# Attention in front of two feed-forward networks: contiguous copies, scores of one head on 64 rows, first fills shared by two engines

## What is computed

```python
scores = scale * np.matmul(q, k.transpose(0, 1, 3, 2))
mask_local = (rel >= 0) & (rel < stride)                       # heads 0 to 3
mask_strided = (rel >= 0) & (pos[None, :] % stride == pos[:, None] % stride)   # heads 4 to 7
scores = np.where(masks, scores, -1e9); scores -= scores.max(-1, keepdims=True)
attn = np.exp(scores); attn /= attn.sum(-1, keepdims=True) + 1e-9
x = np.matmul(attn, v)                                         # then as 2304 x 512
...
for e in range(E):
    out += P[:, e:e + 1] * (np.maximum(x @ w1[e], 0.0) @ w2[e])
...
h = x @ w_in; return np.where(h > 0, h, np.exp(np.minimum(h, 0)) - 1) @ w_out
```

## Time and profile before

| | us |
|---|---|
| median of 3 runs | 2070.46 |
| lowest, highest | 2066.57, 2079.49 |
| the profiled execution | 2081.29 |
| its span | 2079.5 |
| end of attention, where the networks begin to fill PE | 189.8 |

### The profile page before, as it was taken

The page is one execution under the profiler, slowest core; times in us unless marked ns, Lnnn a source line. Parts: engine busy times, 40 slices in busy tenths (PEclk is TensorE's granted clock), DMA queues, the critical chain, the costliest instruction groups (busy, mean ns, idle before and its releaser), DMA issues. The chain is left out here.

```text
span 2079.5 us, 29859 instructions
## 1 busy us (share of the span) xinstructions
PE 2037.2 (98%) x10611; PEld 1841.7 (89%) x10611; DVE 1430.5 (69%) x2456; ACT 931.8 (45%) x1708; POOL 1163.4 (56%) x1519
## 2 busy tenths in 40 slices
PE   6889999999999999999999999999999999999999
PEld 5878999999999999999999998999999999998988
DVE  3664776666666776666666778776666666678876
ACT  5884334333333333333333377533333333477775
POOL 2344665545545565555555657675555554557653
PEclk8997999999999999999999999999999999999999
DMA  7431222212222222222212222322221222222221
GB/s 149 91 76 43 70 62 72 71 62 71 71 62 72 71 61 62 81 61 63 80 61 63 80 61 61 96 77 62 70 73 61 71 72 61 72 67 66 92 71 52
DMA packets 159555, 147.69 MB, mean 71 GB/s; under 512 B 64688, under 2 KB 126384, under 8 KB 159408
## 3 DMA queue, kind: packets, MB, share of 16 engines
q1 hardware_dynamic: 159408, 145.79, 24.3%
HBM read 141.05 MB, written 4.72 MB: 70 GB/s over the span
## 5 line engine op out<-in xcount | busy, mean ns | idle before, releaser
L486 POOL TENSOR_TENSOR w_lo<-w_raw,w_hi 128x256 fp32r<-128x256 f32 x480 | 354.1, 768 | 752.3 <-ACT w_hi L822 752.3
L1088 DVE SCALAR_TENSOR_TENSOR acc<-psum,prob_eps,acc 128x512 f32<-128x512 f32 x516 | 386.9, 750 | 276.0 <-PE psum L695 270.1
L693 PE MATMUL psum<-w_hi,h_hi 128*128 128x512 f32 x1440 | 563.2, 391 | 0.6 <-issue 0.6
L695 PE MATMUL psum<-w_hi,h_lo 128*128 128x512 f32 x1440 | 563.4, 391 | 0.0
L694 PE MATMUL psum<-w_lo,h_hi 128*128 128x512 f32 x1440 | 561.4, 390 | 0.0
L634 PE MATMUL psum<-x_hi_a,w_hi 128*128 128x384 f32 x1296 | 439.2, 339 | 4.1 <-DVE c L1055 3.4
L637 PE MATMUL psum<-x_hi_a,w_lo 128*128 128x384 f32 x1296 | 439.0, 339 | 0.0
L636 PE MATMUL psum<-x_lo_a,w_hi 128*128 128x384 f32 x1296 | 437.6, 338 | 0.0
L479 POOL TENSOR_TENSOR w_lo<-s_tmp,w_hi 128x256 fp32r<-128x256 f32 x480 | 358.3, 777 | 0.0
L695 PEld LDWEIGHTS psum<-w_hi,h_lo 128*128 128x128 f32 x1440 | 270.3, 188 | 58.0
L693 PEld LDWEIGHTS psum<-w_hi,h_hi 128*128 128x128 f32 x1440 | 270.3, 188 | 43.9 <-issue 0.9
(11 more groups left out here) (115 smaller groups left out, 2800.5 us busy)
## 6 DMA issues: line engine op xcount, KB each, us to landing
w_raw<-in_moe_w_dram SPq DMA_DIRECT2D x192, 512.0 KB, 3.6
w_raw<-in_moe_w_in_dram SPq DMA_DIRECT2D x24, 512.0 KB, 3.4
w_raw<-in_moe_w_out_dram SPq DMA_DIRECT2D x24, 512.0 KB, 3.7
v_l<-in_v_dram SPq DMA_DIRECT2D x24, 128.0 KB, 3.5
out_dram<-acc SPq DMA_DIRECT2D x2, 1536.0 KB, 6.8
raw_l_q<-in_q_dram SPq DMA_DIRECT2D x16, 144.0 KB, 3.3
raw_l_k<-in_k_dram SPq DMA_DIRECT2D x16, 144.0 KB, 3.6
raw_s_q<-in_q_dram SPq DMA_DIRECT2D x16, 144.0 KB
```

The costliest lines, as they stand in the source:

```text
L486: pool.tensor_tensor(w2_lo[n % 2][piece], w2_raw[piece], w2_hi[n % 2][piece].bitcast(f32), ALU.subtract).then_inc(w2_lo_s, 1)
L693: pe.matmul(dst, h_hi[:, i, kk, js], w2_hi[s][:, i, :], start=(i == 0), stop=False)
L695: mm = pe.matmul(dst, h_lo[:, i, kk, js], w2_hi[s][:, i, :], start=False, stop=(i == 1))
L1088: ins = dve.scalar_tensor_tensor(a, y, 1.0 if bare else gate_of(n, j), a, ALU.mult, ALU.add)
```

## The change

- `load_qk` of the local heads: two issues for each of q and k instead of four, one for each half of the tokens, all four heads in one. The tokens of a half are now consecutive, so a fill holds 288 neighbouring tokens.
- The transposes of a fill and of a strided context write their columns into PSUM in token order, so with gaps (`fill_ps`, `x_ps`), and the copies out of it are contiguous (`fill_views`, `x_views`). Each fill is one copy, each group has one x copy.
- `kT` loses its zero halves, and its two memsets. Scores: one matmul for each head, on its own 64 partitions, in the order of heads 0, 1, 2, 3; the heads of the lower partitions write bank 0, those of the upper ones bank 1. The two banks now belong to one group, and the scores of g wait for the mask of g-1. The heads stand in the order 0, 2, 1, 3 from the scores to the context (`HEADS`).
- The first eight fills: ACT copies the even ones, DVE the odd ones (`fill_dve`).
- ACT takes one exponential of a column of `ones` before its first wait for a fill, which brings the table of exponentials in.

```diff
-            kT = [sb(f"kT_{kind}", [P, NH // 2, 2, S], f32, att) for kind in "ls"]
+            kT = [sb(f"kT_{kind}", [P, NH // 2, S], f32, att) for kind in "ls"]
...
+        HEADS = (0, 2, 1, 3)
+
         def score_ps(g):
-            return bank(SC + g % 2).rearrange("p (h w) -> p h w", h=NH)
+            return bank(SC, 2).rearrange("p (h w) -> p h w", h=NH)
...
                 for n, src in enumerate((q, k)):
-                    view = src.rearrange("b h (p j) d -> p j b h d", j=run)
-                    for h in range(NH):
-                        sp.dma_start(raw[n][:, :, h * D:(h + 1) * D],
-                                     view[:, :, b, kind * NH + h, :]).then_inc(qk_in[kind][n], 16)
+                    if kind == 0:
+
+                        tokens = src.rearrange("b h (f p j) d -> f p j b h d", f=2, j=run // 2)
+                        for f in range(2):
+                            sp.dma_start(raw[n][:, f * (run // 2):(f + 1) * (run // 2), :]
+                                         .rearrange("p j (h d) -> p j h d", h=NH),
+                                         tokens[f, :, :, b, 0:NH, :]).then_inc(qk_in[kind][n], 16)
+                    else:
+                        tokens = src.rearrange("b h (p j) d -> p j b h d", j=run)
+                        for h in range(NH):
+                            sp.dma_start(raw[n][:, :, h * D:(h + 1) * D],
+                                         tokens[:, :, b, NH + h, :]).then_inc(qk_in[kind][n], 16)
...
-            for m in (kT[0], kT[1]):
-                pool.memset(m[:, :, :, :], 0.0).then_inc(pads_made, 1)
...
+        def fill_views(kind, f):
             which, pair, half = f // 4, (f // 2) % 2, f % 2
             src = bank(FILL + f % 2)[:, 0:FILL_COLS]
+            dst = (qT, kT)[which][kind][:, pair, :]
+            if kind == 0:
+                return dst[:, half * FILL_COLS:(half + 1) * FILL_COLS], src
+            n = FILL_COLS // RES_RUNS
+            return (dst.rearrange("p (a c) -> p a c", a=RES_RUNS)[:, :, half * n:(half + 1) * n],
+                    src.rearrange("p (a c) -> p a c", a=RES_RUNS))
+
+        def fill_read(eng, i):
+
+            if 0 <= i < FILLS and i % 2:
+                eng.wait_ge(fill_dve, i // 2 + 1)
+            elif i >= 0:
+                eng.wait_ge(fill_out, i // 2 + 1 if i < FILLS else i + 1 - FILLS // 2)
+
+        def fill_ps(kind, f, j):
+
+
+            src = bank(FILL + f % 2)[:, 0:FILL_COLS]
+            if kind == 0:
+                return src.rearrange("p (c j) -> p j c", j=L_RUN // 2)[:, j, :]
+            return src.rearrange("p (a j m) -> p j m a", a=RES_RUNS, m=PER_RES)[:, j, :, :]
+
+        def x_ps(g, c):
+
+            cols_c = bank(XT)[:, c * P:c * P + rows_of(g)]
+            return cols_c if g < L_TILES else cols_c.rearrange("p (m r) -> p r m", m=PER_RES)
+
+        def x_views(b, g):
             r = rows_of(g)
+            src = bank(XT)[:, 0:2 * P].rearrange("p (c w) -> p c w", c=2)[:, :, 0:r]
+            if g < L_TILES:
+                return xT[:, 0:2, b * S + g * L_ROWS:b * S + g * L_ROWS + L_ROWS], src
+            r0, n_res = (g - L_TILES) * RES_TILE, r // PER_RES
+            return (xT[:, 2:4, b * S:(b + 1) * S].rearrange("p c (m r) -> p c m r", r=STRIDE)[:, :, :, r0:r0 + n_res],
+                    src.rearrange("p c (m r) -> p c m r", m=PER_RES))
...
-                wait(pe, masked, b * GROUPS + g - (1 if g else 0))
+                wait(pe, masked, b * GROUPS + g)
                 q0, k0 = cols(g)
                 r, w = rows_of(g), keys_of(g)
-                for pair in range(NH // 2):
-                    mm = pe.matmul(score_ps(g)[0:r, 2 * pair:2 * pair + 2, 0:w], qT[kind][:, pair, q0:q0 + r],
-                                   kT[kind][:, pair, :, k0:k0 + w], start=True, stop=True)
+                for i in (0, 2, 1, 3):
+                    pair, o = divmod(HEADS[i], 2)
+                    rows = slice(o * D, (o + 1) * D)
+                    mm = pe.matmul(score_ps(g)[0:r, i, 0:w], qT[kind][rows, pair, q0:q0 + r],
+                                   kT[kind][rows, pair, k0:k0 + w], start=True, stop=True)
...
                 for c in range(2):
-                    mm = pe.transpose(bank(XT)[:, c * P:c * P + r], ctx_n[g % 2][0:r, 2 * c:2 * c + 2, :],
-                                      ident[0:r, 0:r])
+                    mm = pe.transpose(x_ps(g, c), ctx_n[g % 2][0:r, 2 * c:2 * c + 2, :], ident[0:r, 0:r])
...
-            act.wait_ge(pads_made, 2)
-            for f in range(FILLS):
+
+            act.wait_ge(ones_made, 1)
+            act.activation(top_neg[:, :], ones[:, 0:1], ACT.Exp)
+            for f in range(0, FILLS, 2):
                 fill_copy(0, 0, f)
...
+            for f in range(1, FILLS, 2):
+                dve.wait_ge(filled, f + 1)
+                dve.tensor_copy(*fill_views(0, f)).then_inc(fill_dve, 1)
```

More of the change, by code:

```diff
@@ L207, in build @@
         fill_out = sem("fill_out")
+        fill_dve = sem("fill_dve")
         scored = sem("scored")
@@ L509, in _ @@
                         make_t(PHASE[v_] + 1, t)
-        def fill_copies(kind, f):
+        def fill_views(kind, f):
             which, pair, half = f // 4, (f // 2) % 2, f % 2
             src = bank(FILL + f % 2)[:, 0:FILL_COLS]
[L514 to L526, removed]
@@ L528, in x_copies @@
-        def x_copies(b, g):
-            r = rows_of(g)
[L530 to L537, removed]
+            dst = (qT, kT)[which][kind][:, pair, :]
@@ L543, in fill @@
                 if f % (FILLS // 2) == 0:
-                    pe.wait_ge(qk_in[kind][which], (NH * 16) * (b + 1))
+                    pe.wait_ge(qk_in[kind][which], (2, NH)[kind] * 16 * (b + 1))
                 raw, run, rows = ((raw_l, L_RUN, L_ROWS), (raw_s, S_RUN, S_PART))[kind]
-                wait(pe, fill_out, b * (2 * FILLS) + FILLS * kind + f - 1)
+                fill_read(pe, b * (2 * FILLS) + FILLS * kind + f - 2)
                 for j in range(run // 2):
                     jj = half * (run // 2) + j
-                    mm = pe.transpose(bank(FILL + f % 2)[:, j * rows:(j + 1) * rows],
-                                      raw[which][:, jj, 2 * pair * D:(2 * pair + 2) * D],
+                    mm = pe.transpose(fill_ps(kind, f, j), raw[which][:, jj, 2 * pair * D:(2 * pair + 2) * D],
                                       ident[0:rows, 0:rows])
@@ L562, in scores @@
                 if g == 0 or g == L_TILES:
-                    pe.wait_ge(fill_out, b * (2 * FILLS) + FILLS * (kind + 1))
-                wait(pe, masked, b * GROUPS + g - (1 if g else 0))
+                    fill_read(pe, b * (2 * FILLS) + FILLS * (kind + 1) - 2)
+                    fill_read(pe, b * (2 * FILLS) + FILLS * (kind + 1) - 1)
+                wait(pe, masked, b * GROUPS + g)
                 q0, k0 = cols(g)
                 r, w = rows_of(g), keys_of(g)
-                for pair in range(NH // 2):
-                    mm = pe.matmul(score_ps(g)[0:r, 2 * pair:2 * pair + 2, 0:w], qT[kind][:, pair, q0:q0 + r],
-                                   kT[kind][:, pair, :, k0:k0 + w], start=True, stop=True)
+                for i in (0, 2, 1, 3):
[3 more added lines that the diff above has]
+                                   kT[kind][rows, pair, k0:k0 + w], start=True, stop=True)
                 mm.then_inc(scored, 1)
@@ L589, in context @@
                 r, w = rows_of(g), keys_of(g)
-                for h in range(NH):
+                for i, h in enumerate(HEADS):
                     vv = v_l[0:w, g, h, :] if kind == 0 else v_s[0:w, g - L_TILES, h, :]
-                    mm = pe.matmul(bank(CX)[0:r, h * (D + 1):(h + 1) * (D + 1)], probT[g % 2][0:w, h, 0:r], vv,
+                    mm = pe.matmul(bank(CX)[0:r, h * (D + 1):(h + 1) * (D + 1)], probT[g % 2][0:w, i, 0:r], vv,
                                    start=True, stop=True)
@@ L706, in _ @@
             pe.wait_ge(ident_in, 16)
-            pe.wait_ge(pads_made, 4)
+            pe.wait_ge(pads_made, 2)
             for f in range(FILLS):
@@ L771, in fill_copy @@
                 act.wait_ge(filled, b * (2 * FILLS) + FILLS * kind + f + 1)
-                for dst, src in fill_copies(kind, f):
-                    a = act.activation(dst, src, ACT.Copy)
-                a.then_inc(fill_out, 1)
+                act.activation(*fill_views(kind, f), ACT.Copy).then_inc(fill_out, 1)
             def exps(b, g):
@@ L792, in x_copy @@
                 act.wait_ge(ctx_t, n + 1)
-                for dst, src in x_copies(b, g):
-                    a = act.activation(dst, src, ACT.Copy)
-                a.then_inc(x_done, 1)
+                act.activation(*x_views(b, g), ACT.Copy).then_inc(x_done, 1)
             def split_x(p, o):
```

## The result

The changed kernel takes 2088.24 us (median of 14 runs, 2082.3 to 2127.22), the kernel before 2073.81 us beside it. The ratio is 1.0088, 95% interval 1.0066 to 1.0109: slower by about 0.9%, 18 us, where 14 us less had been forecast. The runs spread over 45 us, those of before over 13; the fastest of the changed kernel is slower than the slowest of before.

What follows compares the result with a forecast made beforehand. TensorE, busy 98% of the span, was taken as the bound, with gains possible only in about 190 us of attention. Terms -2.2 - 12 - 3.6 + 4 = -13.8 us gave 2056.5 us, range 2040 to 2080.

Steps and rivals of the forecast that it cites:

- The clock: Attention from batch 1 on: fewer PE stalls make TensorE's clock fall less often, -3.6 us, bounds +4 and -10.
- the clock goes down more often: Rival, attention: less active array or moved stalls mean more steps at 1.2 GHz; seven steps, 15 us, 2072; chance 0.15.
- Scores, +4 us: Score groups on PE: +0.1 us each for entering and leaving the 64-row shape; cases +30, 0, -17 us.
- the two halves side by side: Score groups: upper and lower array halves work in parallel, columns take half, -0.44 us per group, -17 us in all.
- The upper bound, 0.82 + 0.85: Score groups: if weight loads and columns add up, a group costs 1.67 us, +0.8 us each, +30 us in all.
- What is late next is PE itself: Attention after the copies get shorter: PE's own work becomes the limit; 2 of 14.2 us idle left standing.
- Transfers, -2.2 us: SP's queue: four q and k issues instead of eight per batch bring batch 1's q earlier; bounds 0 and -2.7.
- Fill and x copies, -12 us: ACT copies in attention: contiguous fills at 0.40 us and one x copy remove PE's stalls; bounds -8 and -14.
- The start: Before the first score: some 5 us earlier, but swallowed by the stop for q at batch 1; value 0.
- Strided writes: Transposes writing PSUM with gaps, in fills and strided contexts: taken as 0; bounds no cost or two to four times.
- The rival that was to make it slower: Gaps in PSUM slow the fill and strided context transposes; three times as long adds 36 us, 2092; chance 0.12.
- The sum: All terms: -2.2 - 12 - 3.6 + 4 = -13.8 us, forecast 2056.5 us.

Runs made afterwards that it cites:

- experiment 2: The kernel before with only the 64-row scores of the change (one buffer of two banks, one copy per k fill): 2119.69 us, ratio 1.0114.
- full rows: The changed kernel with the scores of before (two matmuls of 128 rows per group, two score buffers): 2058.75 us, ratio to before 0.9927.
- Experiments 1 and 2: The changed kernel with the full-row scores of before, 2058.75 us; the kernel before with only the 64-row scores, 2119.69 us.
- experiments 8 and 10: Every score computed twice: in the changed kernel with next q and k issued before v_s, 2057.78 us; in the changed kernel itself, 2066.1 us.
- experiment 7: The changed kernel with next q and k issued before v_s, score matmuls ordered lower, lower, upper, upper half: 2067.14 us, ratio 1.0003.
- experiment 6: The changed kernel with full-row scores and next q and k issued before v_s, but scores waiting for the previous group's mask: 2052.63 us, ratio 0.9921.

## Why the prediction was wrong

*The clock, the step that failed.* The prediction wrote "With the stalls of 1.4 to 1.9 us gone it should fall less often" and took -3.6 us, bounds +4 and -10. In the profiled executions the lower level cost 16 us more than before, not less, and the kernel with 64-row scores alone has a run that spends the whole of attention there (experiment 2). The term took fewer stops for fewer falls, and never asked whether the shorter score groups would let the clock come back. In the profiles both went wrong: the clock fell at each of the three stops behind 72 us (2.16, 2.68 and 1.35 us), and stayed down for 13.8, 12.3 and 31 us; with full rows no stretch is longer than 14 us. The rival "the clock goes down more often" named the mechanism ("if 64-row scores leave the array less active") with a chance of 0.15, but at seven steps and 15 us. About 29 us of median (2088.2 against 2058.8 with full rows, both in the change), or 33 by the ratios, is the size of all that the new scores do. Experiments 1 and 2 show that the scores are the cause, experiments 8 and 10 that it acts through the clock, since added work takes it away. Not shown is what in the scores does it: the 64 rows, the shorter time or, together with them, the single buffer.

*Scores, +4 us.* Wrong in sign: a group takes 0.64 us instead of 0.93 and its neighbours 0.14 more, some -5 us for 37 groups, between the stated 0 and -17. The +0.1 us for going into the 64-row shape and out again, which rested on no row, was about right; what was missing is that the group itself gets 0.3 us shorter. The prediction's sign for the two halves side by side, a group of 0.6 us, came, but experiment 7 gives the same time with the halves in turn, so what makes the group shorter isn't shown. (The upper bound, 0.82 + 0.85, set the length of a record against a distance from start to start; by the latter the context takes 0.66 us.) The single buffer was put at nothing "unless DVE is late"; DVE is late in batch 3, PE waits 2.4 us for the mask, and the two forms differ by 1.3 us (experiment 6).

*Stops for q.* "What is late next is PE itself", the prediction said; it put no price on the q of batches 2 and 3. Faster steps made it late, 4.8 us, and each such stop began a low stretch. With full rows only 0.24 and 0.54 us of these stops are left, and the clock stays up through both. Moving q ahead of v_s is worth 18 us in the changed kernel, 7 in the kernel before and 7 with full rows (by the ratios 20, 10 and 3).

*Transfers, -2.2 us.* Nothing: two issues of q take 1.58 us at the start and of k 2.55, the masks behind them 1.42 instead of 0.63, and SP reaches the weights 0.25 us later. The reason given for the gain failed too: at batch 1 the last q issue ends 1.4 us earlier than before (37.18 instead of 38.62 us), since the second weight issue got shorter, and q lands at the same time all the same. The bound of 0 was right.

*Fill and x copies, -12 us.* Right in what they do. ACT by line and shape in the changed kernel, beside the earlier trace rows:

```profile
L814 ACT ACTIVATE xT<-psum 128x252 f32<-128x252 f32 x16 | 6.4, 400 | 6.3 <-PE psum L626 6.3
L795 ACT ACTIVATE kT_s<-psum 128x288 f32<-128x288 f32 x16 | 5.9, 406 | 1.9 <-PE psum L571 1.8
```

0.406 us against the forecast 0.40, and PE no longer waits for xT (11.9 us before, under 1 now). In place of it came 8.9 us of other idleness, so of 12 us only 5 stayed. With full rows 5.8 us of idleness are left of 14.2, and 8 stayed, the smallest gain within the bounds.

*The start.* First score 4.2 us earlier, forecast 5, and swallowed by the stop for q as said: the fill of batch 1 begins at 42.56 after 42.62.

*Strided writes.* No cost: the six transposes of two local fills take 0.49 us from start to start at the upper level before and after (84.73 to 85.22, 127.06 to 127.55). A transpose stands as one record, unlike the other fp32 matmuls. The rival that was to make it slower did not happen. The Trainium skill (SBUF — State Buffer, the note on cachelines) lets one expect that matmuls slow down significantly; this trace has 96 columns written 12 bytes apart and shows nothing of it.

*The sum* for all but the scores looks right: with full rows the ratio gives -15 us, forecast -14. Part of that is luck. In the profiles of before and of the kernel with full rows, from 42.6 us on, idleness makes -8.5 us where the copies were to make -12, the clock -14.7 instead of -3.6, and the +4 for the scores and the -2.2 for the transfers have no part in it. The profile of before is one of its slower runs, which is why these two add up to more than 15.

## What to carry to other kernels

A stage of many short matmuls can lose more to TensorE's clock than a faster matmul gives back: before an edit shortens PE's work in such a stage, find in the profile where the clock falls, how many steps it takes to come back, and put the price on the recovery. Test it by doing the shortened work twice; if the kernel gets faster, the work was not what cost time, and the lengths of records before and after show what part of it was the clock. Look at every stop and at the start before you say how soon the clock comes back: at one stop here it took 9 to 10 us in three kernels, with full rows, with 64 rows and with 64 rows twice. And ask of each step that gets quicker which transfer it will now arrive too early for: moving the issues of q ahead of twenty small ones was worth 3 to 20 us.

## What the runs showed of the hardware

- TensorE can be busy without a gap for 100 us and stay at 1.2 GHz (experiment 2, 50 to 150 us). The Trainium skill (TensorE: Matmul & The Clock Gate, the table "Why this matters for your kernels") advises to keep TensorE busy continuously to get the full clock. This trace disagrees for short fp32 matmuls and transposes: here busy in the profile wasn't enough.
- One run of the kernel before with 64-row scores took 3736 us, another 2271. Most of that can't lie in attention, which ends by 240 us in the profiled run of this kernel. These two have no profile; the record gives a mean granted clock of 0.83 for both, 0.965 or more for the others. Where the rest of the time went isn't shown.
- A record of a 64-row fp32 matmul with 128 columns takes 0.077 us at the upper level (0.61 / 8), one of a full-row matmul with 256 columns 0.22 (0.87 / 4). For the same columns the 64-row form is 30% shorter, in either order of the halves. Going into the 64-row shape and out of it costs about 0.14 us at the upper level, which falls on the neighbours: 0.08 to 0.10 on the operation ahead (0.84 to 0.91, 0.50 to 0.60), 0.06 on the one behind (0.33 to 0.39). It is the same with 8, 12 and 16 records in a group, so it is paid once for a group. The Trainium skill (TensorEngine Tiling, "Key Properties") says that a change of tiling mode drains TensorE; these traces agree with such a cost.
